# One unit's scale moved from pair 0 to pair 1, one square moved behind a second cast, and three table reads gathered at the top of a loop

## What is computed

```python
logits = x @ w_gate                      # 3072 x 8
expert_idx = np.argmax(logits, axis=1)
...
for e in range(E):
    mask = expert_idx == e
    xe = x[mask]
    h = np.maximum(xe @ w1[e], 0.0)      # 320 -> 1024
    ye = h @ w2[e]                       # 1024 -> 320
    out[mask] = gate_w[mask, None] * ye
```

## Time and profile before

| | |
|---|---|
| time, median of 3 runs | 812.52 us (811.38 to 813.29) |
| the profiled execution | 810.98 us |
| its span | 808.9 us, of which 235 to 447 us is the loop over pairs |
| PE busy | 743.7 us, 92% of the span |
| DVE, ACT, POOL busy | 517.6, 416.1 and 197.5 us |
| mean granted TensorE clock | 0.98 |

### The profile page before, as it was taken

The page is one execution under the profiler, slowest core; times in us unless marked ns, Lnnn a source line. Parts: engine busy times, 40 slices in busy tenths (PEclk is TensorE's granted clock), DMA queues, the critical chain, the costliest instruction groups (busy, mean ns, idle before and its releaser), DMA issues.

```text
span 808.9 us, 18071 instructions
## 1 busy us (share of the span) xinstructions
PE 743.7 (92%) x6472; PEld 551.0 (68%) x6473; DVE 517.6 (64%) x1352; ACT 416.1 (51%) x811; POOL 197.5 (24%) x287
## 2 busy tenths in 40 slices
PE   3899999996687999989999899999999999999994
PEld 3687898884476887878888755566565555565552
DVE  6768899998786557654687655455465455554441
ACT  4577777767753557535674233343433433434332
POOL 4477787784322001101010000020100100100101
PEclk9999999998699999999999999999999999999998
DMA  6879979760627956958220000000000000000000
GB/s 192 222 220 305 322 218 341 211 194 24 192 81 243 384 185 227 311 209 283 83 83 1 2 2 1 1 34 1 21 13 1 32 0 0 32 0 0 34 1 32
DMA packets 39517, 95.87 MB, mean 119 GB/s; under 512 B 7150, under 2 KB 19630, under 8 KB 39438
## 3 DMA queue, kind: packets, MB, share of 16 engines
q1 hardware_dynamic: 31010, 66.33, 26.2%
q10 hardware_dynamic: 5788, 19.47, 6.7%
q0 software_dynamic: 2640, 9.01, 3.3%
HBM read 70.92 MB, written 23.89 MB: 117 GB/s over the span
## 4 chain that ended last, share of the span: by engine, by line
PE 79%; DVE 8%; DMA 4%; issue 4%; ACT 2%; SPq 1%; POOL 1%; DVEq 0%; ACTq 0%; POOLq 0%
PE bank L1762 33%; PE bank L1912 19%; PE bank L1796 11%; PE bank L1623 4%; PE bank L1647 4%; PE bank L1633 1%; PE bank L1669 1%; PE bank L1639 1%; PE bank L1752 1%; DMA slot<-qkT 1%; DMA d_x<-og 1%; PE bank L1613 1%; PE bank L1889 1%; PE bank L1615 1%; ACT slot L797 1%
## 5 line engine op out<-in xcount | busy, mean ns | idle before, releaser
L1762 PE MATMUL bank<-stage,slot 128*128 128x512 f16 x768 | 181.1, 379 | 0.0
L1912 PE MATMUL bank<-slot,dec 128*128 128x320 f16 x768 | 159.1, 299 | 0.0
L1762 PE MATMUL bank<-qbd,slot 128*128 128x128 f16 x1984 | 117.8, 221 | 11.7 <-issue 10.2
L1762 PEld LDWEIGHTS bank<-stage,slot 128*128 128x128 f16 x768 | 75.1, 98 | 74.3 <-DVE stage L1555 0.2
L1762 PEld LDWEIGHTS bank<-qbd,slot 128*128 128x128 f16 x1984 | 113.8, 99 | 15.2 <-issue 14.6
L1559 DVE TENSOR_TENSOR qk<-stage,dec 128x512 f16<-128x512 f32 x96 | 66.5, 692 | 84.6 <-ACT dec L1004 84.6
L1912 PE MATMUL bank<-slot,qk 128*128 128x320 f16 x384 | 114.8, 299 | 0.0
L713 POOL DMA_INDIRECT out<-stage,tok_i x24 | 23.7, 986 | 366.8 <-ACT stage L1015 362.8
L1004 ACT CAST dec<-stage 128x512 f16<-128x512 f32 x96 | 59.5, 620 | 100.5 <-PE bank L1912 74.3
L1555 DVE TENSOR_TENSOR stage<-bank,stage 128x512 f32<-128x512 f32 x96 | 66.2, 690 | 67.5 <-ACT stage L998 66.5
L998 ACT ACTIVATE stage<-bank 128x512 f32<-128x512 f32 x96 | 57.3, 597 | 97.6 <-PE bank L1762 96.6
(11 more groups left out here) (275 smaller groups left out, 1197.3 us busy)
## 6 DMA issues: line engine op xcount, KB each, us to landing
slot<-d_w SPq DMA_DIRECT2D x12, 1280.0 KB, 8.0
stage<-wB SPq DMA_DIRECT2D x6, 1280.0 KB
d_w<-slot ACTq DMA_DIRECT2D x6, 1280.0 KB, 7.3
stage<-wA SPq DMA_DIRECT2D x6, 1024.0 KB, 6.0
d_w<-slot SPq DMA_DIRECT2D x4, 1280.0 KB, 8.2
stage<-wB ACTq DMA_DIRECT2D x4, 1280.0 KB
qk<-qkT SPq DMA_DIRECT2D x12, 360.0 KB, 5.9
slot<-qkT SPq DMA_DIRECT2D x12, 360.0 KB, 8.0
```

The source lines that it names most:

```text
L1762: ins = t_.matmul(pf, a[:, col:col + P], x(k), start=(q == 0), stop=(q == len(ops) - 1))
L1912: ins = t_.matmul(bank[4 + q][:, 0:DM], x[f % 2][:, q * P:(q + 1) * P], slotB[2 + f // NF][:, c0:c0 + DM], start=(f == 0 and z == 0), stop ...
```

## The change

On ScalarE, square(5, 2) moves from between x_high(0, 0) and x_high(1, 1) to behind the latter. On VectorE, scale(5) moves from pair 0 (between x_scale(3) and the low parts of unit 4) to pair 1 (between x_scale(4) and the low parts of unit 4 there). On TensorE, the wait for the first link of that scale moves from before h_product of pair 2 to before y_product of pair 1. In the loops, the three experts that two pairs need (of pairs p-1, p and p+1) are read at the top of the turn, where each of the two pairs read two before.

```diff
@@ scalar, ahead of the pairs
             x_cast(0, 0)
             x_cast(1, 1)
             x_high(0, 0)
-            square(5, 2)
             x_high(1, 1)
-            for k in range(3, NSL):
+            for k in range(2, NSL):
                 square(5, k)
@@ vector
             h_low(0, 0)
             x_scale(3, 1)
-            scale(5)
             jobs(0)
             gates()
             x_low(2, 0)
...
                 if p + 3 < NPAIR:
                     x_scale(p + 3, 1 - i)
+                if p == 1:
+                    scale(NS)
                 if p in PAIR_SCALE:
                     scale(PAIR_SCALE[p])
@@ tensor
                     with pe.Fori(lo, lo + n, 2) as p:
+                        e = [expert(p + i) for i in range(-1, 2)]
                         for i in range(2):
-                            pair(p + i, (lo + i) % 2)
+                            pair(p + i, (lo + i) % 2, e[i + 1], e[i])
                 if lo + n < hi:
-                    pair(hi - 1, (hi - 1) % 2)
-
-            def pair(p, i, unit=None):
-                now, before = expert(p), expert(p - 1)
+                    pair(hi - 1, (hi - 1) % 2, expert(hi - 1), expert(hi - 2))
+
+            def pair(p, i, now, before, unit=None):
                 h_product(p, i, now)
...
             y_product(0, 0, expert(0))
             x_turn(3, 1)
+            after = expert(1)
+            h_product(2, 0, expert(2))
             pe.wait_ge(sc_chain, scaled(NS) - SC_UNIT + 1)
-            pair(2, 0)
+            y_product(1, 1, after)
+            x_turn(4, 0)
             at = 3
             for p in sorted(PAIR_SCALE):
                 pairs(at, p)
-                pair(p, p % 2, PAIR_SCALE[p])
+                pair(p, p % 2, expert(p), expert(p - 1), PAIR_SCALE[p])
                 at = p + 1
```

## The result

The changed kernel takes 822.26 us (median of 4 runs, 818.63 to 825.21) against 812.03 (4 runs, 811.38 to 813.29): a ratio of 1.0122, 95% interval 1.0077 to 1.0167. A second measurement gave 818.53 against 810.26, 1.0119 (1.0081 to 1.0156). So the direction was right, and the size was not: 822.26 lies above the range (815.0 to 821.5), and the +6.85 us forecast stands against +10.2 and +8.3 measured.

The account below looks back on a forecast made before the run. TensorE was taken to set the end of every pair. Terms 1.6 - 0.5 - 0.8 + 5.9 + 0.65 = +6.85 us on the 812.52 us median gave 819.4, taken as 819.0 us; range 815.0 to 821.5.

Parts of the forecast that it names:

- The reads: Tops of pairs 5, 7, 10, 16, 18, 20, 25, 27: third read costs +0.7 or +0.75 us each, +5.9 in all.
- Pair 6: Two slow reads leave the middle of a turn, so the issue idle time before this pair goes: -0.8 us.
- pair 10: One of the loop tops: a third read in a chain without slack, +0.75 us.
- pair 14: Loop top where y_product(13)'s 0.59 us wait for VectorE behind h_product takes the delay up: 0.
- Pair 23: Loop top with some slack left, so the third read costs +0.65 us.
- Pair 3: Slow third read 1.35 us plus VectorE's 0.25 us before this pair: +1.6 us, bounds +1.0 and +1.9.
- The scale's microsecond: Moved scale starts h_product(2) about 1.0 us earlier; gone by pair 3, as x_turn(4) waits for x_low(3, 1).
- Pair 4: 2.39 us stall inside h_product: the sequencer comes to it sooner, -0.5 us, bounds 0 and -0.6.
- the clock: Rival: longer gap before pair 3 lowers TensorE's granted clock there, +1.6 us more, 820.6 us; chance 0.1.
- The rival of the deeper queue: Rival: sequencer's lead grows to 3.6 us, reads at tops hide; -1.05 us, or 811.5 us; chance 0.1.

Follow-up runs that it names:

- a_reads: Kernel before with only the expert reads gathered at the top of the loop, scale, wait and square unmoved: 821.13 us against 811.87, ratio 1.0116.
- e_split: Changed kernel with its three reads split, two at the top of a turn and the third between its two pairs: 811.88 us, 0.9991 of the kernel before.
- d_fourth: Changed kernel with a fourth read at each top, its value unused: 826.92 us, 1.0209 of the kernel before.
- b_front: Changed kernel with the old loop and its two reads before each pair; scale, wait and square moved alone: 810.42 us, 0.9994 of the kernel before.
- c_square: Kernel before with only square(5, 2) moved behind x_high(1, 1): 811.01 us against 811.87, ratio 0.9984.
- j_after: Changed kernel measured once more without an edit: 818.53 us against 810.26 for the kernel before, ratio 1.0119.
- g_filler: Changed kernel with 14 matmuls of unused result behind x_turn(4), before pair 3: 820.34 us, 1.0100 of the kernel before.
- i_fill_tops: Changed kernel with 14 unused matmuls before pair 3 and three at each top ahead of the reads: 821.70 us, 1.0099 of the kernel before.
- h_carry_front: Changed kernel's scale, wait and square, with one read per pair issued before x_turn's wait and carried in two registers: 800.90 us, 0.9861 of the kernel before.
- f_carry: Kernel before with one read per pair, issued before x_turn's wait and carried between turns in two registers: 803.30 us against 812.06, ratio 0.9871.

## Why the prediction was right in its direction and too small

**The reads, right.** The step "at a top there is a third read in a chain without slack" holds: at the tops of pairs 5, 7, 18, 20, 25 and 27 the third read costs 0.67, 0.65, 0.65, 0.66, 0.72 and 0.67 us by the starts of the timeline (0.70 to 0.75 was forecast), at pair 16 0.70 together with what stands ahead of it. a_reads shows that it is the reads, e_split that it is their place, d_fourth that a further one costs the same again. Pair 6 gave its 0.8 us.

**Tops that came out otherwise.** At pair 10 the forecast was +0.75 and the profile has -0.20: before, the sequencer was only 1.1 us ahead there, after 2.0. The 0.71 us of idle time before pair 10 is of that one execution: b_front and c_square, with the old reads, have none and reach pair 10 0.87 us sooner. Against those two the third read costs 0.67 us here too; the forecast compared with an execution that was late at this place. At pair 14 VectorE's wait took up 0.42 of 0.61 us and not all. Pair 23 is +0.54 for +0.65.

**Pair 3, right but for the clock.** The scale's microsecond was gone by pair 3 as the prediction said, because x_turn(4) waits for x_low(3, 1): from h_product(0) to h_product(3) it is 1.5 us more (1.6 was forecast), with three slow reads of 0.89 to 1.24 us. b_front shows the same for the scale alone. h_product(0) itself ran at half clock in this execution (4.78 us from its first to its last matmul, for 3.59), but that is not in the 1.5: h_low(0) starts only 0.2 us later, measured from h_product(0), and x_low(3, 1) hangs on h_low(0).

**Pair 4, wrong.** The -0.5 us did not come: 2.42 us are left of 2.39 (2.03 in the second profile). The stall goes with a fetch of code, below.

**The term that was mis-sized: the clock.** This is the step that failed. The prediction had it as a rival with chance 0.1 and +1.6 us, "with pair 3's gap growing". The sum itself put the clock at nothing. In the profile h_product(3) has 1.55 us more from the half clock, h_product(4) 1.2 and y_product(3) some 0.4: 3.2 us that the sum did not have. The part of h_product(4) behind its stall, before and after (39 and 37 matmuls):

```profile
255.51 2.34 PE bank L1762 x39
```

```profile
259.58 3.51 PE bank L1762 x37
```

The gap before pair 3 was known to grow to about 4 us; what was not drawn from it is that half clock there was the likely case (after, j_after and d_fourth have it) and that more than one pair can pay. By the clock's records in the traces, the time at half clock from h_product(2) to h_product(30) is 10.2 us in after, j_after, a_reads and g_filler and 13.7 in d_fourth, 6.8 in i_fill_tops, but 3.4 or none in all seven kernels without the three gathered reads. Over whole runs the mean clock goes the same way: 0.970 to 0.973 for every kernel with the reads gathered at the tops and no filling work, 0.975 to 0.981 for every kernel without. That mean also counts what lies ahead of the pairs, though (before h_product(0) 23.8 us at half clock in before, 31.5 in after, 17.1 in j_after), and so it does not show the size of the term by itself.

**The sum.** Forecast 6.85. By the profile: pair 3 +1.5, clock +3.2, tops +5.3 (5, 7, 10, 14, 16, 18, 20, 23, 25, 27), pair 6 -0.8, the last pairs and pair 13 +0.5, start of the first pair +0.9, which is ahead of the changed instructions of the pairs and differs from one execution to the next. Together 10.6 at the start of h_product(30), with an execution that is 10.3 longer in all. Without the clock and the start it is 6.5, against the forecast's 6.85. That these two lie so near is in part luck: the tops gave 5.3 for a forecast of 6.55, and pair 4's -0.5 that did not come and the last pairs' +0.5 make up for most of it.

**The rival of the deeper queue, wrong.** By the lead of x_turn in the middle pairs, 2.2 to 2.4 us after as before, the lead is capped, though the middle of a turn has no reads any more. The 64 instructions of the Trainium skill ("Advanced Engine Details and Errata", Engine Queue Depths) are not borne out for this stream: 2.2 to 2.4 us behind y_product's matmuls are at most 36 instructions, and the 0.99 us behind h_product's are 36 again.

## What to carry to other kernels

Where a sequencer works ahead of an engine by a fixed number of instructions, a table read is free only as long as the whole chain between two stretches of engine work fits into that lead; a loop's top, which has its own branch, is the last place to gather reads. Read one turn early, carry the value in a register, and put the read before a wait and not behind it: here the three together were worth 8.8 us, and saving a read without moving the others nothing. When an edit lengthens an idle stretch of TensorE, price the clock too, and read a kernel's small pieces of idle time from more than one profile.

## What was not expected of the hardware

**A read's price depends on other traffic.** It takes 0.30 us as a rule and up to 1.34 us behind a store of weights. All the slow ones in the loops (0.4 us and more) start within 10 us of the issue of such a store, as the three before pair 3 do (0.89 to 1.24 us), though not every read there is slow: in before the two at 363 us, 5 us behind a store, take 0.30. Beside loads of weights alone it stays fast: before pair 8 the two reads of before take 0.31 and 0.30 us, in a stretch (280 to 284.5 us) with the DMA engines busy throughout (share 1.02).

**The stall inside h_product(4) goes with a fetch of code.** In before, after, j_after, a_reads, b_front, c_square and e_split one packet of the instruction queue starts within 0.3 us of the last matmul ahead of the stall (in after at 257.2 us; the row is from the view of DMA queues over 257 to 260 us: packets, MB, share).

```profile
q8 instruction: 1, 0.02, 2.0%
```

And it moves with the code: after 25 of 64 matmuls in before, b_front and c_square, 26 in e_split, 27 in after, j_after and a_reads, 28 in h_carry_front, 29 in f_carry, as instructions come and go ahead of it; in g_filler, with 14 matmuls put ahead of the loop, after 13. In f_carry and h_carry_front the packet starts 0.9 and 1.3 us ahead of the stall, which is then 1.3 and 1.1 us long from matmul to matmul, for 2.6; in g_filler it starts 1.0 us behind, and the stall is 3.4 us long. So the stall ends 2.2 to 2.4 us behind the start of the packet in all twelve profiles that have one. In d_fourth a packet starts at 256.8 us, in the middle of h_product(4), and there is no stall; why, no run shows.

The Trainium skill has a rule near this ("Runtime: NRT & Kernel Launch", Instruction fetch mechanics): a taken branch to code outside the blocks at hand has to wait for a DMA fetch. The trace agrees in the blocks, 49 packets of that queue carrying 0.80 MB, 16 KB each. That it is this rule is not shown: the branch ahead of the stall (L1781, at 251.2 us in before) takes 0.2 us, and the stall comes 25 matmuls behind it. By these profiles a few instructions more or less ahead of a loop go with up to 2.6 us, once, with no change to the work.
